# Attention of 32 heads in fp32: queries and keys split on GpSimd ahead of the transposes, and query halves exchanged by DMA

## What is computed

```python
def _attn_ref(q, k, v, s):          # 4 batches, 8 heads, 576 positions, 64 columns
    scores = scale * np.matmul(q, k.transpose(0, 1, 3, 2))
    cum = np.cumsum(np.maximum(s, 0.0), axis=-1)
    bias = -(cum[:, :, :, None] - cum[:, :, None, :])
    scores = np.where(causal, -1000000000.0, scores + np.minimum(bias, 0.0))
    attn = np.exp(scores - np.max(scores, axis=-1, keepdims=True))
    attn = attn / (np.sum(attn, axis=-1, keepdims=True) + 1e-09)
    return np.matmul(attn, v)
def _moe_ref(x, g_ln, w_ch1, w_ch2):  # after attention; then _moe2_ref, which mixes tokens first
    return x + np.maximum(norm(x) * g_ln @ w_ch1, 0.0) @ w_ch2
```

## Time and profile before

| | |
|---|---|
| time before, median of 3 runs | 1120.89 us (1119.97 to 1123.44) |
| the profiled execution | 1120.59 us, span 1118.7 us |
| TensorE, VectorE, ScalarE, GpSimd busy over the span | 94%, 72%, 49%, 30% |
| 160 to 200 us (attention): TensorE, VectorE, ScalarE, GpSimd busy | 34.60, 37.11, 34.76, 7.64 us of 40.00 |
| mean granted clock of TensorE | 0.992 |

### The profile page before, as it was taken

How to read it: one execution, slowest core, us unless ns; L and a number is a source line. 1 busy time by engine, 2 the same in 40 slices (tenths; PEclk the granted TensorE clock), 3 DMA queues, 4 the chain that set the end, 5 groups by cost and what they waited for, 6 DMA issues and landing times.

```text
span 1118.7 us, 20942 instructions
## 1 busy us (share of the span) xinstructions
PE 1056.2 (94%) x6936; PEld 930.6 (83%) x6936; DVE 802.1 (72%) x1712; ACT 545.7 (49%) x1245; POOL 338.2 (30%) x375
## 2 busy tenths in 40 slices
PE   6888888888797999999999999999999999999998
PEld 5777777776687899889899888888988988888887
DVE  6999999999558668667667667875865766765533
ACT  5888888888333344244344334433423432423321
POOL 1244212117214433333324232343332323232100
PEclk9999999999799999999999999999999999999999
DMA  6655454465242221312231343422142233223131
GB/s 158 163 134 120 123 134 118 125 175 165 86 138 85 83 75 59 128 59 76 76 113 58 113 151 102 158 99 95 57 132 94 76 94 114 80 91 113 58 124 46
DMA packets 157475, 118.85 MB, mean 106 GB/s; under 512 B 87712, under 2 KB 132768, under 8 KB 157408
## 3 DMA queue, kind: packets, MB, share of 16 engines
q1 hardware_dynamic: 157408, 117.95, 35.6%
HBM read 98.97 MB, written 18.95 MB: 105 GB/s over the span
## 4 chain that ended last, share of the span: by engine, by line
PE 91%; ACT 3%; DVE 2%; issue 2%; POOL 1%; DMA 1%; ACTq 0%; SPq 0%; DVEq 0%; POOLq 0%
PE ps_up L746 10%; PE ps_up L748 9%; PE ps_up L747 9%; PE ps_acc L793 7%; PE ps_acc L792 6%; PE ps_acc L794 6%; PE ps_s L793 5%; PE ps_s L792 5%; PE ps_s L794 5%; PE ps_x L676 5%; PE ps_s L646 4%; PE ps_pt L657 3%; ACT prob L922 2%; PE ps_up L657 2%; PE ps_up L622 2%
## 5 line engine op out<-in xcount | busy, mean ns | idle before, releaser
L746 PE MATMUL ps_up<-z,w 128*128 128x256 f32 x896 | 257.2, 287 | 3.8 <-DVE z L1253 3.8
L748 PE MATMUL ps_up<-z,w 128*128 128x256 f32 x896 | 254.2, 284 | 0.0
L747 PE MATMUL ps_up<-z,w 128*128 128x256 f32 x896 | 254.2, 284 | 0.0
L556 POOL TENSOR_TENSOR w_f<-raw 128x256 f32<-128x256 f32 x64 | 71.2, 1113 | 413.2 <-DMA raw<-in_moe_w_ch 390.1
L746 PEld LDWEIGHTS ps_up<-z,w 128*128 128x128 f32 x896 | 171.9, 192 | 10.4 <-DVE z L1253 4.3
L747 PEld LDWEIGHTS ps_up<-z,w 128*128 128x128 f32 x896 | 172.1, 192 | 6.1 <-issue 1.2
L748 PEld LDWEIGHTS ps_up<-z,w 128*128 128x128 f32 x896 | 172.5, 192 | 0.0
L792 PE MATMUL ps_acc<-w_hi,h 128*128 128x512 f32 x320 | 126.9, 396 | 2.1 <-DVE x_res L1279 2.1
L793 PE MATMUL ps_acc<-w_lo,h 128*128 128x512 f32 x320 | 126.8, 396 | 0.0
L794 PE MATMUL ps_acc<-w_hi,h 128*128 128x512 f32 x320 | 126.2, 394 | 0.0
L1074 ACT ACTIVATE h<-ps_up 128x256 fp32r<-128x256 f32 x64 | 24.5, 383 | 185.4 <-PE ps_up L748 185.4
(11 more groups left out here) (160 smaller groups left out, 2619.3 us busy)
## 6 DMA issues: line engine op xcount, KB each, us to landing
raw<-in_moe_w_ch SPq DMA_DIRECT2D x80, 512.0 KB, 3.6
ncum_b<-ncum_dram SPq DMA_DIRECT2D x32, 288.0 KB, 3.6
x_in<-x_dram SPq DMA_DIRECT2D x18, 512.0 KB, 4.5
k_raw<-in_k SPq DMA_DIRECT2D x64, 128.0 KB, 2.5
u_dram<-x_in SPq DMA_DIRECT2D x9, 512.0 KB, 2.8
q_raw<-in_q SPq DMA_DIRECT2D x32, 128.0 KB, 3.2
v_raw<-in_v SPq DMA_DIRECT2D x32, 128.0 KB, 2.2
w_f<-in_moe_w_ch SPq DMA_DIRECT2D x4, 1024.0 KB, 6.7
```

The source lines that it names most:

```text
L556: pool.tensor_tensor(to[:, I5, 1], a21, a22, ALU.add).then_inc(s1_done, 1)
L746: nc.tensor.matmul(bank, w_hi, z_hi, start=(start and c == 0), stop=False, skip_group_check=True)
L747: nc.tensor.matmul(bank, w_hi, z_lo, start=False, stop=False, skip_group_check=True)
L748: last = nc.tensor.matmul(bank, w_lo, z_hi, start=False, stop=(stop and c == 1), skip_group_check=True)
```

## The change

Queries, keys and last rows are split by GpSimd in SBUF before TensorE transposes them (`split_rows`): each row then holds its 64 high and its 64 low parts side by side, so that one transpose puts the high parts on partitions 0 to 63 and the low parts on 64 to 127. ScalarE (`copy_q`) and VectorE (`copy_k`, `copy_last`) copy each bank out of PSUM once. Two passes of `scores` need the query once as it is and once with its halves exchanged; SyncE makes the exchanged copy by four more DMAs per head, from SBUF to SBUF (`swap_queries`, `swap_last`). Keys are loaded once, in the layout of the queries, last rows once. The sums of a head are inverted by GpSimd, with an addition and a `pow`, in place of VectorE. The second weight matrix is loaded whole after the first two heads, and split one slice a head in heads 4 to 19. New small tiles hold constants; `SP_PAD` columns of `q_swap` are zeroed at the start. `split_keys` and `split_last` are like `split_queries`, with their own tiles and semaphores.

```diff
@@ sync: loads, and two exchanges
             def load_q(u):
 
-                wait(sp, qt_done, u)
+                wait(sp, q_lo_done, u)
                 sp.dma_start(q_raw[:], flat_rows(q_f, u)).then_inc(q_loaded, 16)
 
             def load_k(u):
-                wait(sp, kt_done, u)
-                for a in range(2):
-                    sp.dma_start(k_raw[:, :, a], whole_tiles(k_f, u)).then_inc(k_loaded, 16)
+                wait(sp, k_lo_done, u)
+                sp.dma_start(k_raw[:], flat_rows(k_f, u)).then_inc(k_loaded, 16)
 
             def load_last(u):
-                waits_apart(sp, (lt_done, u))
+                waits_apart(sp, (l_lo_done, u))
                 for flat, to in ((q_f, slice(0, LAST)), (k_f, slice(LAST, P))):
-                    sp.dma_start(last_raw[to], last_tile(flat, u).unsqueeze(1).to_broadcast([LAST, 2, D])).then_inc(last_loaded, 16)
+                    sp.dma_start(last_raw[to, 0], last_tile(flat, u)).then_inc(last_loaded, 16)
+
+            def swap_queries(u, p):
+
+                waits_apart(sp, (q_done, u + 1))
+                for to, of in ((slice(0, D), slice(D, P)), (slice(D, P), slice(0, D))):
+                    sp.dma_start(q_swap[p][to, 0:FULL].bitcast(F32), qk[p][of, 0, 0:FULL].bitcast(F32)).then_inc(q_swapped[p], 16)
+
+            def swap_last(u, p):
+                waits_apart(sp, (l_done, u + 1))
...
                 if exists(u + 3):
                     load_q(u + 3)
+                if exists(u + 1):
+                    swap_last(u + 1, 1 - p)
+                if exists(u + 2):
+                    swap_queries(u + 2, p)
                 if not first:
                     store_head(*before(m, p))
                 if exists(u + 3):
@@ sync: prologue
             load_q(2)
             load_k(2)
+            for p in range(2):
+                swap_queries(p, p)
+            swap_last(0, 0)
...
             head_alone(0, 0, first=True)
             load_second(0)
+            load_second(KC)
             head_alone(0, 1)
-            load_second(KC)
-            with sp.Fori(1, LAST_M - 2) as m:
+            load_second(2 * KC)
+            load_second(3 * KC)
+            with sp.Fori(1, LAST_M - 1) as m:
                 head_alone(m, 0)
                 head_alone(m, 1)
-            head_alone(LAST_M - 2, 0)
-            load_second(2 * KC)
-            head_alone(LAST_M - 2, 1)
-            load_second(3 * KC)
@@ gpsimd
+            def split_rows(u, x, split, loaded, transposed, hi_done, lo_done):
+
+                pool.wait_ge(*loaded)
+                waits_apart(pool, (transposed, u))
+                pool.tensor_tensor(split[:, :, 0, :], x[:], one[:].unsqueeze(2).to_broadcast(x.shape), ALU.mult).then_inc(hi_done, 1)
+                pool.wait_ge(hi_done, u + 1)
+                pool.tensor_tensor(split[:, :, 1, :], x[:], split[:, :, 0, :].bitcast(F32), ALU.subtract).then_inc(lo_done, 1)
+
+            def split_queries(u):
+                split_rows(u, q_raw, q_split, (q_loaded, 16 * u + 16), qt_done, q_hi_done, q_lo_done)
...
+            def invert_sums(u):
+
+                p = u % 2
+                pool.wait_ge(exp_done, QT * u + QT)
+                waits_apart(pool, (x_head_done, u - 1))
+                pool.tensor_tensor(inv_sum[:, p], row_sum[:, p], epsilon[:], ALU.add).then_inc(sum_eps_done, 1)
+                pool.wait_ge(sum_eps_done, u + 1)
+                pool.tensor_tensor(inv_sum[:, p], inv_sum[:, p], minus_one[:], ALU.pow).then_inc(inv_done, 1)
...
             pool.wait_ge(pads_done, 1)
-            for u in range(4):
+            for u in range(HEADS):
+                if u + 2 < HEADS:
+                    split_queries(u + 2)
+                if u > 0:
+                    invert_sums(u - 1)
                 split_values(u)
-            for j in range(2 * KC):
-                split_values(4 + j)
-                split_second(j)
...
+                if u + 2 < HEADS:
+                    split_keys(u + 2)
+                    split_last(u + 2)
+                if 4 <= u < 4 + JC:
+                    split_second(u - 4)
+            invert_sums(HEADS - 1)
             inverse_root(0)
@@ tensor
+            def transpose_rows(bank, split):
+
+                to = bank.rearrange("d (n t) -> d t n", t=QT - 1)
+                for t in range(QT - 1):
+                    last = nc.tensor.transpose(to[:, t], twice(split[:, t]).bitcast(F32), ident)
+                return last
+
             def transpose_q(m, p):
                 u = 2 * m + p
 
-                waits_apart(pe, (q_loaded, 16 * u + 16), (l_lo_done, u))
...
+                waits_apart(pe, (q_lo_done, u + 1), (l_done, u))
+                transpose_rows(up[0], q_split).then_inc(qt_done, 1)
...
             def transpose_k(m, p):
                 u = 2 * m + p
-                pe.wait_ge(k_loaded, 32 * u + 32)
+                pe.wait_ge(k_lo_done, u + 1)
...
                 if i == 0:
-                    pe.wait_ge(q_lo_done, u + 1)
-                    pe.wait_ge(k_lo_done, u + 1)
-                    pe.wait_ge(l_lo_done, u + 1)
+                    pe.wait_ge(q_done, u + 1)
+                    pe.wait_ge(k_done, u + 1)
+                    pe.wait_ge(l_done, u + 1)
+                    pe.wait_ge(q_swapped[p], 32 * (m + 1))
+                if i == QT - 1:
+                    pe.wait_ge(l_swapped[p], 32 * (m + 1))
...
-                    for n, kk in enumerate((k_hi, k_lo)):
-                        last = nc.tensor.matmul(bank, q2[:, i * P:(i + 1) * P], kk[:, lo:hi], start=(n == 0), stop=(n == 1 and not diag))
+                    for n, qq in enumerate((qk[p][:, 0], q_swap[p][:])):
+                        last = nc.tensor.matmul(bank, qq[:, i * P:(i + 1) * P], qk[p][:, 1, lo:hi], start=(n == 0), stop=(n == 1 and not diag))
@@ scalar: q_high, k_high and last_high go, copy_q stands where q_high stood
+            def copy_q(m, p):
                 act.wait_ge(qt_done, 2 * m + p + 1)
-                nc.scalar.activation(q2s[p][0:D, 0:FULL], up[0][0:D, 0:FULL], ACT.Copy, scale=-SCALE).then_inc(q_hi_done, 1)
...
+                nc.scalar.activation(qk[p][:, 0, 0:FULL], up[0][:, 0:FULL], ACT.Copy, scale=-SCALE).then_inc(q_done, 1)
@@ vector: q_low, k_low, last_low and invert_sums go, copy_k and copy_last stand where k_low and last_low stood
+            def copy_k(m, p):
+                dve.wait_ge(kt_done, 2 * m + p + 1)
+                nc.vector.tensor_copy(qk[p][:, 1, 0:FULL], k_bank(2 * m + p)[:, 0:FULL]).then_inc(k_done, 1)
+
+            def copy_last(m, p):
+                dve.wait_ge(lt_done, 2 * m + p + 1)
+                nc.vector.tensor_tensor(qk[p][:, :, FULL:S], up[0][:, 0:P].rearrange("p (a n) -> p a n", a=2),
+                                        last_scale[:].unsqueeze(2).to_broadcast([P, 2, LAST]), ALU.mult).then_inc(l_done, 1)
```

More of the change, by code:

```diff
@@ L161, in chain_kernel @@
             prob_2_0 = sbuf("prob_2_0", [P, FULL], F32, small)
-            q2s = [sbuf(f"q2{p}", [P, SP_PAD], F32R, small) for p in range(2)]
+            q_swap = [sbuf(f"q_swap{p}", [P, SP_PAD], F32R, small) for p in range(2)]
             prob_3 = sbuf("prob_3", [P, FULL], F32, small)
@@ L226, in chain_kernel @@
         l_hi_done, l_lo_done = sem("l_hi_done"), sem("l_lo_done")
+        q_done, k_done, l_done = sem("q_done"), sem("k_done"), sem("l_done")
+        q_swapped, l_swapped = [sem(f"q_swapped{p}") for p in range(2)], [sem(f"l_swapped{p}") for p in range(2)]
         v_hi_done, v_split = sem("v_hi_done"), sem("v_split")
@@ L610, in transpose_q @@
-                for t in range(QT - 1):
-                    last = nc.tensor.transpose(bank[:, t], q_raw[:, t], ident)
-                last.then_inc(qt_done, 1)
+                waits_apart(pe, (q_lo_done, u + 1), (l_done, u))
+                transpose_rows(up[0], q_split).then_inc(qt_done, 1)
             def transpose_k(m, p):
                 u = 2 * m + p
-                pe.wait_ge(k_loaded, 32 * u + 32)
+                pe.wait_ge(k_lo_done, u + 1)
                 if not (isinstance(u, int) and u == 0):
-                    pe.wait_ge(q_lo_done, u + 1)
@@ L942, in head_alone @@
                 probs_high(m, p, 1)
-                if not final:
-                    last_high(*after(m, p))
                 exponential(m, p, 3)
@@ L949, in head_alone @@
                 if more:
-                    q_high(*second(m, p))
+                    copy_q(*second(m, p))
                 if final:
@@ L960, in head_alone @@
                 probs_high(m, p, 4)
-                if more:
-                    k_high(*second(m, p))
                 if not final:
@@ L1171, in head_alone @@
                 bias_and_max(m, p, 3)
-                if not first:
-                    invert_sums(*before(m, p))
                 if not final:
-                    last_low(*after(m, p))
+                    copy_last(*after(m, p))
                 probs_low(m, p, 1)
@@ L1184, in head_alone @@
                     weights_low(0)
```

(2 more changed lines are left out.)

106 lines of the change are left out of this document (42 added, 64 removed).

## The result

| | before | changed |
|---|---|---|
| time, median on the same chip | 1121.05 us (1119.97 to 1123.44) | 1176.84 us (1175.28 to 1177.58) |
| ratio | 1 | 1.0481, 95% interval 1.0462 to 1.0500 |
| span of the profiled execution | 1118.7 us | 1173.5 us |
| mean granted clock of TensorE | 0.992 | 0.990 |

A forecast was written before the change was run, and what follows sets the result against it. TensorE's own chain was taken to bound the kernel, VectorE not. On 1120.6 us, the new loop through GpSimd and SyncE adds 68, start 5, bursts 2, end minus 1.5: 1194 us, range 1155 to 1236.

The forecast's parts named there:

- `pow`: GpSimd's `pow` over 5 columns in the inversion of the sums: 1.7 us taken, between ends of 1.13 and 2.5.
- the circle: Loop through GpSimd's and SyncE's queues, from values via the queries' load to the next values: 10.8 us a head, 68 us added.
- Two signs: In attention: chain of waits through GpSimd's split, landing of `q_raw` and SyncE; TensorE waits for the split keys.
- the second circle: Loop through the exchange of the last rows and the scores of tile 4: 9.6 us a head, hidden behind 10.8.
- The landing: Queries' load, issue to landing: 3.3 us from the trace, 2.9 to 3.7; by the skill's page an estimate of 2.3 us.
- TensorE's transposes of the queries: In each head, 128 columns cost what the keys cost: 0.15 us more, hidden where TensorE's chain waits.
- GpSimd's keys, last rows and weights: Splits behind the values, about 1.4, 0.6 and 2.4 us: costed at nothing, covered by the landing of the queries.
- 8.8 us of issues: SyncE's issues per head: 7.2 us now and some 1.6 more, inside the loop's 10.8 but above 8.36.
- Start and bursts: Later first scores and keys of head 1: 5 us, 3 to 8; second weight matrix in two 2 MB bursts: 2 us, 0 to 5.
- The end: End of attention: GpSimd's inverse root starts at about 281.2, no weight slices ahead; 1.5 us won, from 0 to 3.
- under 75%: Sign in attention: VectorE's busy share falls below 75%.
- the rival: In attention, TensorE's granted clock falls from 2.4 to 1.2 GHz as it idles more: 1313 us; chance 0.06.

The follow-up runs named there:

- the run with both circles open: Changed kernel with the load of the queries and the exchange of the last rows both ahead of the values in SyncE's order; 1150.65 us, ratio 1.0237.
- the reordered kernels: Changed kernel with queries' load and all four exchanges ahead of the values: 1153.41 us; with inversion on VectorE besides: 1152.51; with that and the exponential of tile 4 earlier: 1152.18.
- the reordered kernel: Changed kernel with queries' load and all four exchanges ahead of the values, inversion on VectorE; 1152.51 us, ratio 1.0257; with the exponential of tile 4 earlier 1152.18 us, 1.0260.

## Why the prediction was right, and where its sizes were off

**The sign and the circle: right.** The forecast was that the order "values split, SyncE's loads, landing of the queries, split, inversion, values" closes on itself. It does, head after head, and moving that load ahead of the values undoes 17 us by itself. Two signs that the forecast named did not come: the chain of waits goes through the exchange and not through the landing of `q_raw`, and TensorE does not wait for the split keys in the heads from 60 to 300 us. Both come from the second circle being nearly as long as the first.

**The length of the circle: 9.96 us in place of 10.8.** The mean of 10.11 over 28 heads holds the long one; without it the circle adds 28 x (9.96 - 8.36) = 45 us, where 68 was forecast, and the period lies at the lower end of the 10 to 12 us that were named as the sign. Term by term for the head shown, which is 10.34 us long, forecast and measured: values 1.67 and 1.66; until SyncE issues 0.21 and 0.24; to the load of the queries 2.04 and 1.98; landing and start 3.51 and 3.67; split 1.43 and 1.38; addition 0.28 and 0.28; `pow` 1.7 and 1.13 until the values start. The term that was off is `pow`: between the bounds 1.13 and 2.5 I chose 1.7, and the lower one is what holds. From 2 columns to 5 it hardly grows. That is 0.57 of the 0.88 us (10.84 less 9.96), 16 of the 23 us a run. Most of the rest is the landing, which is longer in the head shown than in the mean (3.37 us with the start), and the way to the load of the queries (1.92).

**The landing.** The landing of the trace, 3.3 us, held: 3.2 in the median. The runs with the load in front of values and bias row give 2.0 to 2.1. So here the difference goes with the load's place in SyncE's order. The Trainium skill, "DMA: Bandwidth & Descriptors" (Anatomy of one DMA), states its fit of 2.0 us and the bytes over 436 GB/s for DMAs that GpSimd issues, which the forecast did not say; these come from SyncE. The estimate of 2.3 us by it is 0.9 below the measured landing at the place of the forecast, and 0.2 to 0.3 above it in front.

**The second circle: called hidden, and it was, by 0.4 us.** I had put it at 9.6 us against 10.8; it is 9.95 against 10.34 in the head shown. Its landing was the wrong term, 2.86 us for the 2.2 that I took from a load of the last rows; the way from the queries' load to the second exchange's issue was 1.0 for 1.4, and tile 4 took 2.17 for 2.04. The gap of 1.2 us that I forecast would have let a shorter first circle pay; at 0.4 it did not, as the inversion on VectorE shows: 1.4 us out of the first circle, 0.17 off the mean head.

**TensorE's transposes of the queries: forecast 0.15 us a head more, measured none.** Four of them take 0.60 us in TensorE's timeline in both kernels, with 64 columns before and with 128 after. It would have made no difference to the time, since TensorE waits elsewhere in the head.

**GpSimd's keys, last rows and weights: nothing, as forecast.** They end 1.4 us before the queries arrive. The forecast also said what they cost without that cover, 9.5 us a head in the sixteen heads with slices; with `pow` at its measured length this is 8.9, and the run with both circles open shows 8.86. The expectation of that run used this number, and its miss lies elsewhere, in SyncE.

**SyncE: 8.8 us of issues, called covered by the circle, and they are.** Where the circles are opened, they measure 9.19 us a head, and that is the floor that the reordered kernels show, 23 us over 28 heads above the 8.36 before. The forecast had seen that this term is above 8.36, and a change of SyncE's order takes none of its issues away.

**Start and bursts: 11.4 us for 5 + 2.** Head 1 comes 7.4 us later, and the burst adds 4.0 us more in the long head. Part of the 7.4 goes with the bursts too: with the loads spread, head 1 comes 2.3 us earlier. So the whole forecast was 19 us too long as a circle too long by 23 and a start and bursts too short by 4: the sum is a little closer than its largest term, by luck. The end: 1.7 us given back for 1.5. GpSimd's last inversion and the root in the chain of waits of the changed kernel:

```profile
336.22 0.70 POOL inv_sum L584
...
337.00 1.55 POOL inv_sum L586
338.55 0.68 POOL rstd L598
```

The root ends at 339.23, and no slices of the weights stand ahead of it now.

**VectorE: 68% where under 75% was forecast.** The inversion, moved alone, is worth nothing in two kernels; the low parts of queries and keys were not moved alone. **The clock:** the rival did not come true in the changed kernel. It came up in runs that were meant to be faster.

## What to carry to other kernels

When work moves to an engine that shares one-deep buffers with an in-order DMA queue, write down the circle "release, issue, landing, work, release" and add up its terms: its sum is a floor for the period, however idle the engines are. Add up the queue's own time for its issues as well: with both circles open, it was the next floor here. Look for the second circle before opening the first, and compare the start of the gated instruction with the end of its engine's own work, because a chain of waits can name the circle that has a little slack. The best gain here came from none of this: it was one exponential issued ahead of a copy, at the only wait that the chain of the kernel before showed.

## What the runs showed of the hardware

- `pow` on GpSimd costs nearly the same over 5 columns and over 2 (1.18 and 1.13 us), so it is nearly all fixed cost at these sizes.
- Thirteen DMA issues a head take SyncE 9.19 us when it waits for nobody: 6.38 us of issues and 2.81 between them.
- The landing of the same 128 KB load depends on its place: 3.2 us behind the values and the bias row, 3.8 with the exchange of the last rows moved ahead, 2.0 in front of them all. What it shares its time with was not measured.
- The granted clock fell behind two waits of TensorE that stood next to each other (1.08 and 0.59 us in one run, 0.95 and 1.17 in another). That this is the cause is not shown: the early exponential in the reordered kernel shortened the first of the two to 0.4 us, and the mean clock stayed at 0.976. In the changed kernel TensorE is busy for 0.25 us in the window from 172 to 174 and the clock stays full:

```profile
172.00:174.00 2.00, 0.25 (x3) 0.01 (x1) 1.71 (x6) 1.91 (x6) 0.58 (x2) 1.00 0.69 193
```

After 0.49 of 2.00 us in the reordered kernel it stood at 0.50 for 6 us. What tells these two places apart was not found out.
- The inversion at the end of the attention took longer than in the loop, 0.70 and 1.55 us for 0.20 and 1.17 (rows above). No run looked for the cause.
